# Turning the down-sampled probabilities on VectorE in 32x32 blocks instead of on TensorE

## The reference, cut to what matters

```python
q_d, k_d, v_d = (a.reshape(B, H, S // 4, 4, D).mean(axis=3) for a in (q, k, v))   # B 4, H 8, S 576, D 64
out_d = softmax(scale * q_d @ k_d.T) @ v_d            # 144 queries x 144 keys for each head
out_up = np.repeat(out_d, 4, axis=2)
scores = np.where(abs(i - j) < 4, scale * q @ k.T, -1e9)
x = out_up + softmax(scores) @ v                      # (2304, 512)
x = ((x @ w1) * (x @ w2)) @ w3 @ w_out                # 512 -> 1024 -> 512
out = max(x @ u1, x @ u2, x @ u3) @ u_out             # 512 -> 768 -> 512
```

## Time and profile before

| | |
|---|---|
| median of 3 runs | 675.64 us (674.79 to 677.38) |
| the profiled execution | 676.02 us, its span 673.8 us |
| PE busy | 668.0 us (99%), weight loads 641.4 us (95%) |
| DVE, ACT, POOL busy | 406.6 us (60%), 268.5 us (40%), 354.8 us (53%) |
| DMA | 178.14 MB, 264 GB/s on average |
| granted TensorE clock | full (1.00) |

### The profile page before, as it was taken

The page is one execution under the profiler, slowest core; times in us unless marked ns, Lnnn a source line. Parts: engine busy times, 40 slices in busy tenths (PEclk is TensorE's granted clock), DMA queues, the critical chain, the costliest instruction groups (busy, mean ns, idle before and its releaser), DMA issues.

```text
span 673.8 us, 15807 instructions
## 1 busy us (share of the span) xinstructions
PE 668.0 (99%) x6272; PEld 641.4 (95%) x6272; DVE 406.6 (60%) x779; ACT 268.5 (40%) x590; POOL 354.8 (53%) x375
## 2 busy tenths in 40 slices
PE   9999999999999999999999999999999999999998
PEld 8878989999998999999999999999999999999997
DVE  5465666656655754376444564676676766757673
ACT  5565434534434344466545562222431223312230
POOL 5999668866994244464345442233761235803341
PEclk9999999999999999999999999999999999999999
DMA  9795479899857759778999698978399773997632
GB/s 303 267 312 162 126 208 290 256 275 280 239 152 236 237 201 385 265 229 318 323 359 357 240 349 320 415 287 299 115 395 340 236 259 129 353 382 228 243 110 94
DMA packets 93240, 178.14 MB, mean 264 GB/s; under 512 B 8560, under 2 KB 40560, under 8 KB 92400
## 3 DMA queue, kind: packets, MB, share of 16 engines
q1 hardware_dynamic: 93168, 177.15, 76.9%
HBM read 135.69 MB, written 41.42 MB: 263 GB/s over the span
## 4 chain that ended last, share of the span: by engine, by line
PE 98%; DVE 1%; issue 0%; ACT 0%; DVEq 0%
PE psum L966 30%; PE psum L968 29%; PE psum L967 29%; PE psum L1011 3%; PE psum L976 2%; PE psum L1020 2%; PE psum L999 1%; PE psum L984 1%; PE psum L1096 1%; PE psum L989 1%; ACT psum L1548 0%; PE psum L1032 0%; DVE gate L1340 0%; PE psum L1035 0%; PE psum L1038 0%
## 5 line engine op out<-in xcount | busy, mean ns | idle before, releaser
L1769 POOL TENSOR_TENSOR second_split<-xy,second_split 128x384 fp32r<-128x384 f32 x99 | 104.1, 1071 | 153.4 <-ACT second_split L1543 153.4
L966 PE MATMUL psum<-second_split,weights_split 128*128 128x384 f32 x402 | 134.7, 335 | 0.0
L967 PE MATMUL psum<-second_split,weights_split 128*128 128x384 f32 x402 | 134.3, 334 | 0.0
L968 PE MATMUL psum<-second_split,weights_split 128*128 128x384 f32 x402 | 134.3, 334 | 0.0
L966 PE MATMUL psum<-weights_split 128*128 128x384 f32 x278 | 93.5, 336 | 0.0
L968 PE MATMUL psum<-weights_split 128*128 128x384 f32 x278 | 92.9, 334 | 0.0
L967 PE MATMUL psum<-weights_split 128*128 128x384 f32 x278 | 92.9, 334 | 0.0
L1769 POOL TENSOR_TENSOR weights_split<-xy,weights_split 128x384 fp32r<-128x384 f32 (+1 forms) x64 | 72.7, 1155 | 16.4 <-ACT weights_split L1543 16.3
L966 PEld LDWEIGHTS psum<-second_split,weights_split 128*128 128x128 f32 x402 | 75.4, 188 | 0.7 <-ACT sums L1543 0.3
L967 PEld LDWEIGHTS psum<-second_split,weights_split 128*128 128x128 f32 x402 | 75.5, 188 | 0.0
L968 PEld LDWEIGHTS psum<-second_split,weights_split 128*128 128x128 f32 x402 | 75.5, 188 | 0.0
(11 more groups left out here) (157 smaller groups left out, 1410.6 us busy)
## 6 DMA issues: line engine op xcount, KB each, us to landing
weights_split<-weights_stream SPq DMA_DIRECT2D x39, 768.0 KB, 5.4
weights_split<-weights_stream SPq DMA_DIRECT2D x54, 512.0 KB, 7.3
weights_split<-gate_weights_stream SPq DMA_DIRECT2D x105, 256.0 KB, 4.8
weights_stream<-attention SPq DMA_DIRECT2D x48, 256.0 KB, 3.8
xy<-wa SPq DMA_DIRECT2D x40, 256.0 KB, 5.1
weights_stream<-attention SPq DMA_DIRECT2D x24, 384.0 KB, 3.6
weights_split<-weights_stream SPq DMA_DIRECT2D x6, 1152.0 KB, 5.0
attention<-v_win SPq DMA_DIRECT2D x16, 384.0 KB, 4.7
```

What stands on the lines that cost most here:

```text
L966: pe.matmul(out, lhs[:, 0], rhs[:, 0], start=first, stop=False, skip_group_check=read_between)
L967: pe.matmul(out, lhs[:, 0], rhs[:, 1], start=False, stop=False, skip_group_check=read_between)
L968: return pe.matmul(out, lhs[:, 1], rhs[:, 0], start=False, stop=last, skip_group_check=read_between)
L1769: return pool.tensor_tensor(out, full, high.bitcast(F32), ALU.subtract)
```

## The change

The T visit, ScalarE's copy of the turned tiles and the identity are gone. `scale_down` normalises the probabilities in place in PSUM, and VectorE then transposes them in 32x32 blocks into SBUF (128 x 480: three groups of queries, the 144 keys padded to 160). A block transpose leaves the queries of partition group 32i in partition group 32i, so each of the four groups of 32 partitions (two heads, two halves of 24 queries in each group of 48) has its keys in blocks of 32 rows. The values are then 20 matmuls (five key blocks, two heads, two halves) of 32 keys x 64 by 72 queries, each half into a bank of its own, instead of four of 72 x 64 by 144. v is laid out in DRAM in blocks of 32 keys and twice, once for each half: 128 partitions with 1280 numbers each instead of 80 with 1024. The sum over four rows covers 128 partitions, 640 and then 320 numbers. `copy_up` is two copies, one for each head. `qk_sum` no longer waits for the turned probabilities of the unit before, since its buffer is no longer shared.

```diff
-DJ, DROWS, DSTEP, DOWN = 3, 64, 40, 48
+DJ, DAHEAD, DSTEP, DOWN, DROWS = 3, 8, 48, 24, 64
+DB = -(-SD // TW)
+SD_PAD = DB * TW
...
-VISITS = {"S": 0, "T": 5, "V": 7.6}
+VISITS = {"S": 0, "V": 7.6}
...
-        v4_in_sb = cut(2 * FACTOR * P, TD_PAD).rearrange("p (k j c) -> p k j c", k=2, j=FACTOR)
-        v4_sb = v4_in_sb[0:TD]
-        vd = cut(2 * P, TD).rearrange("p (k c) -> p k c", k=2)
+        v4_sb = cut(DB * FACTOR * D).rearrange("p (b j c) -> p b j c", b=DB, j=FACTOR)
+        vd = cut(DB * D).rearrange("p (b c) -> p b c", b=DB)
...
+        def pv_down(h):
+            banks = psum[:, 512 * (4 + 2 * h):512 * (6 + 2 * h)].rearrange("p (n c) -> p n c", n=2)
+            return banks[D * h:D * (h + 1), :, PV_DOWN:PV_DOWN + DJ * DOWN]
...
-            def turns(u):
-                pe.wait_ge(down_scaled, u + 1)
...
-                for kt in range(2):
-                    for j in range(DJ):
-                        mm = pe.transpose(turned_d[:, kt, P * j:P * (j + 1)], prob_d[:, j, TD * kt:TD * (kt + 1)], ident)
-                mm.then_inc(down_turned, 1)
...
             def values(u):
...
-                pe.wait_ge(turn_copied, u + 1)
...
                 pe.wait_ge(vd_ready, u + 1)
-                for kt in range(2):
+                pe.wait_ge(down_turned, u + 1)
+                for b in range(DB):
                     for h in range(2):
-                        first = DJ * P * kt + D * h
-                        own = prob_dt_all[:, first:first + 136 * DJ].rearrange("p (j c) -> p j c", j=DJ)[:, :, 0:DOWN]
-                        mm = pe.matmul(pv_down[D * h:D * (h + 1), :], vd[:, kt, D * h:D * (h + 1)], own,
-                                       start=kt == 0, stop=kt == 1)
+                        for half in range(2):
+                            first = D * h + TW * half
+                            rows = slice(first, first + min(TW, SD - TW * b))
+                            mm = pe.matmul(pv_down(h)[:, half, :], vd[rows, b, :], own_rows(rows, b, half),
+                                           start=b == 0, stop=b == DB - 1)
...
-                ge(dve, down_turned, u)
+                ge(dve, down_scored, u)
...
-                dve.tensor_tensor(prob_d, score_d, drc.unsqueeze(2).to_broadcast([P, DJ, SD]),
+                dve.tensor_tensor(score_d, score_d, drc.unsqueeze(2).to_broadcast([P, DJ, SD]),
                                   ALU.mult).then_inc(down_scaled, 1)
+                if u == 0:
+                    dve.wait_ge(zeros_made, 4)
+                ge(dve, down_filled, u)
+                dve.wait_ge(down_scaled, u + 1)
+                dve.transpose(prob_d, score_d_all).then_inc(down_turned, 1)
...
-            def copy_turned(u):
-                act.wait_ge(down_turned, u + 1)
-                copy(prob_dt, turned_d).then_inc(turn_copied, 1)
...
-                copy(up_t, pv_down).then_inc(up_ready, 1)
+                for h in range(2):
+                    up = copy(up_t.rearrange("p (j n c) -> p n j c", j=DJ, n=2)[D * h:D * (h + 1)],
+                              pv_down(h).rearrange("p n (j c) -> p n j c", j=DJ))
+                up.then_inc(up_ready, 1)
```

More of the change, by code:

```diff
@@ L151, in position @@
     if u < PAIRS:
-        late = {"v_sum": 3.7 if u == 0 else 3.5, "copy_turned": 0.8}.get(name, late)
+        late = {"v_sum": 3.7 if u == 0 else 3.5}.get(name, late)
         if name == "copy_up" and u == 0:
@@ L526, in build, with own_rows @@
         v_sb = cut(TG * P).rearrange("p (g c) -> p g c", g=TG)
[L527 to L529 removed]
+        v4_sb = cut(DB * FACTOR * D).rearrange("p (b j c) -> p b j c", b=DB, j=FACTOR)
+        vd = cut(DB * D).rearrange("p (b c) -> p b c", b=DB)
         prob_t = cut(2 * TG * TW)
[L532 to L537 removed]
+        ahead_of_q = cut(DAHEAD)
+        q_at = used[0]
+        qkd = cut(2 * SD).rearrange("p (a s) -> p a s", a=2)
+        prob_d_at = used[0]
+        prob_d = cut(DJ * SD_PAD)
+        def own_rows(rows, b, half):
+            at = prob_d_at + TW * b + (0 if half else DAHEAD)
+            return att[rows, at:at + DJ * SD_PAD].rearrange("p (j c) -> p j c", j=DJ)[:, :, 0:DOWN]
         up_t = cut(SD)
         mask = cut(TG * TW).rearrange("p (g k) -> p g k", g=TG)
[L540 removed]
         dnb, dsum, drc = (cut(DJ) for _ in range(3))
         lmax, lrc = (cut(2 * TG) for _ in range(2))
[L544 removed]
+        score_d_all = bank(6)[:, 0:DJ * SD_PAD]
+        score_d_pad = score_d_all.rearrange("p (j k) -> p j k", j=DJ)[:, :, SD:SD_PAD]
+        score_d = score_d_all.rearrange("p (j k) -> p j k", j=DJ)[:, :, 0:SD]
         score_by_head = psum[:, 512 * 4:512 * 6].rearrange("p (h c) -> p h c", h=2)[:, :, 0:TG * TW].rearrange(
@@ L571, in prob_of @@
                 "p (h g q) -> p h g q", h=2, g=TG)
-        turned_d = psum[0:TD, 512 * 6:512 * 8].rearrange("p (k c) -> p k c", k=2)[:, :, 0:DJ * P]
-        pv_down = bank(6)[:, 0:SD]
-        PV = 256
-        dmax, dsum_eps = (bank(6)[:, DJ * (SD + i):DJ * (SD + i + 1)] for i in range(2))
+        PV, PV_DOWN = 256, 400
+        def pv_down(h):
+            banks = psum[:, 512 * (4 + 2 * h):512 * (6 + 2 * h)].rearrange("p (n c) -> p n c", n=2)
+            return banks[D * h:D * (h + 1), :, PV_DOWN:PV_DOWN + DJ * DOWN]
+        dmax, dsum_eps = (bank(6)[:, DJ * (SD_PAD + i):DJ * (SD_PAD + i + 1)] for i in range(2))
         lsum, lsum_eps = (bank(4)[:, 400 + 2 * TG * i:400 + 2 * TG * (i + 1)] for i in range(2))
@@ L975, in scores @@
                         rows = slice(D * h, D * h + D)
-                        mm = pe.matmul(score_d[rows, j, :], qkd[rows, 0, DSTEP * j:DSTEP * j + DROWS], qkd[rows, 1, :],
+                        at = q_at + DSTEP * j - DAHEAD
+                        mm = pe.matmul(score_d[rows, j, :], att[rows, at:at + DROWS], qkd[rows, 1, :],
                                        start=True, stop=True)
@@ L1177, in gated_need @@
                 return 4 * (GP * s + GP - 1) + {0: 0, 6: 1, 7: 3}[i]
-            for step in in_order(pieces_of_product(), parts_of_mlp(), gated_parts(), unit_jobs("STV")):
+            for step in in_order(pieces_of_product(), parts_of_mlp(), gated_parts(), unit_jobs("SV")):
                 if step[0] == "W3O":
@@ L1183, in _ @@
                     scores(step[1])
-                elif step[0] == "T":
-                    turns(step[1])
                 elif step[0] == "V":
@@ L1695, in gated_y @@
                 copy(y_place(s + 1, j, n), bank(G_BANKS[j])[:, 0:HALF]).then_inc(y_ready, 1)
-            run = {"exp_down": exp_down, "exp_local": exp_local, "copy_turned": copy_turned, "copy_up": copy_up,
+            run = {"exp_down": exp_down, "exp_local": exp_local, "copy_up": copy_up,
                    "SPLIT": split_w, "W3O_OUT": product_high, "SPLIT_X": split_x, "GATE": gate_copy, "H": h_high,
@@ L1700, in _ @@
                    "HIGH_WC": high_wc, "XE": split_xs, "K": keep, "G": gated_high, "GY": gated_y}
-            for step in in_order(unit_jobs(["exp_down", "exp_local", "copy_turned", "copy_up"]), weight_splits(),
+            for step in in_order(unit_jobs(["exp_down", "exp_local", "copy_up"]), weight_splits(),
                                  product_out(), x_splits(), after_parts(["GATE", "H", "Y"]),
@@ L1868, in constants @@
         mask[TW * (t % TI):TW * (t % TI + 1), t // TI, :][off < FACTOR] = 0.0
-    return np.eye(P, dtype=np.float32), mask
+    return mask
 def layouts(i):
```

37 lines of the change are left out of this document (14 added, 23 removed), and 2 rows, old and new, of the table FOLLOWS.

## The result

The changed kernel took 681.68 us in the median of 20 runs (677.88 to 691.19, and one outlier), the kernel before 676.46 (674.79 to 679.70): a ratio of 1.0072, 95% interval 1.0051 to 1.0092. Profiled once more beside the experiments (run *again*) it gave 1.0064, 1.0028 to 1.0100. The forecast was 668.1, range 664.2 to 673.5. The kernel before spreads over 5 us, this one over 13.

The account below looks back on a forecast made before the run. PE, busy 99% of the span, was taken as the bound. Prologue 1.8, unit 4 0.66, unit 5 1.03, units 6-9 2.64, 10-12 0.5, 13-14 1.32, unit 15 -0.42, V visits 0: 7.5 us, median 675.64 to 668.1, range 664.2 to 673.5.

Parts of the forecast that it names:

- T visit removed, 0.66 us a unit: PE, between S and V: dropping the T visit saves 0.66 us in each of sixteen units, 10.6 us if all realised.
- V visit, 0.0: PE, down-sampled values in V: 40 records in ten rounds of four cost net 0.0 us a unit, range -0.1 to +0.57.
- the second rival: V visit: the narrow parts do not overlap, +0.57 us in each of 16 units, 677.2 us; chance 0.09.
- VectorE +0.70: New block transpose ahead of scale_local: 0.70 us, 0.76 with the wait; V of unit 5 starts about 95.42, not 94.89.
- the wait near 235: Unit 15: PE waits about 1.0 us on VectorE, times in the old trace; the unit gives -0.42 us.
- POOL +0.42 us: POOL's sum of v grows to 640 and 320 elements, 1.56 and 0.87 us: 0.42 us more a unit.
- The deadline near 62: Units 2 and 3: POOL's v sum is ready at about 62.4, PE waits 0.7 us; prologue gives 1.8 us, not 2.64.
- The one near 190: Units 10 to 12: PE waits 1.4 us for POOL's low part of h; they give 0.5 us, not 1.98.
- The sum, 7.5 us: Whole kernel: gains of the prologue and units 4 to 15 together, taking the median from 675.64 to 668.1 us.
- the part on the queues: ScalarE and DMA queues: 5 MB more for v delays nothing PE waits for; 0, at worst 1 us in the prologue.
- The slower rival: Instruction supply: an "issue" stall of 1 us in every V visit, 16 us more, 684 us; chance 0.06.
- "I expect no change" of the clock: Granted clock stays as it was; the prediction text given here states no size for it.

Follow-up runs that it names:

- fewer_bytes_sooner: Changed kernel with v_down's transfer cut from 640 to 320 KB a unit after the first, and load_qk 1.5 steps sooner: ratio 0.9975, median 675.21 us.
- qk_sooner: Changed kernel with load_qk of each unit 1.5 steps earlier in SyncE's list: ratio 1.0017.
- shift_sooner: Changed kernel with 35 matmuls of 8 columns ahead of V's in unit 4 and load_qk 1.5 steps sooner; its own ratio is not in the text.
- v_later_qk_sooner: Changed kernel with load_v4 behind V in SyncE's list and load_qk 1.5 steps sooner: ratio 1.0053.
- v_later: Changed kernel with load_v4 behind V in SyncE's list (1.2 steps after V's place, not 1.35 ahead): ratio 1.0097.
- fewer_bytes: Changed kernel with v_down's transfer cut from 640 to 320 KB a unit after the first, instructions kept: ratio 1.0024.

## Why the prediction was wrong, point by point

- **T visit removed, 0.66 us a unit: right.** S to V of unit 6 is 10.21 us, 101.42 to 111.63, where it was 10.89.
- **V visit, 0.0: right.** 1.74 us against 1.72. The matmuls on different parts overlap; the second rival is out.
- **VectorE +0.70: right** (0.682). V of unit 5 waited 0.5 us for the transpose, as its forecast start (95.42 for 94.89) implies, and the wait near 235 for L1391 was 0.9 of the forecast 1.0.
- **POOL +0.42 us: right** (1.566 and 0.872 us). The deadline near 62 never showed. The one near 190 does not show in *again*, where PE was late by other losses, but where those were smaller PE waited for POOL's `h_split` there: 1.2 us in fewer_bytes_sooner, 1.0 in qk_sooner and shift_sooner, 0.9 in v_later_qk_sooner, of the forecast 1.4.
- **The sum, 7.5 us: right as far as it went.** Without the three losses the spans are 664 to 666, from 672.7: 6 to 9 us.
- **The step that failed** is in the part on the queues, "Since PE waited for no piece, I take 0, and at worst 1 us in the prologue", with what the sum then left at nothing: that PE's instructions and the clock stay as they are. The 5 MB were priced by mean bandwidth, and wrongly: at 264 GB/s, 1.2 us is the price of 320 KB, one unit; 5.24 MB take 19.8 us of the DMA engines. That is no loss by itself, but it is not small. In place of the 0 stand 11.0 us more of gaps at portion ends, 4.5 us of waits for x_out and 5.1 us of the clock in *again*. What was lost is delay: of the portion's packet, 3.3 us after the request for 2.5, and of qk. Moving v_down behind V took the gaps of units 5 to 12 away (v_later). How much of it is the bytes and how much the place of the transfer is open.
- **The slower rival named the right mechanism and was given 0.06.** It had one row for it, the 0.8 us in L984 of unit 14. It counted "such a stall in every V visit" and set against it that there was one in 32. The row's place would have said more: that gap stands at instruction 6849, 193 more than a multiple of 256. From there the number of instructions a unit, 455 to 508, and with it where the ends would fall, could have been worked out. It is 0.5 to 3.3 us in seven places, not 1 us in 16, and in S and dense work rather than in V.
- **"I expect no change" of the clock: wrong.** It cost 5.1 us in *again* and nothing in the two fastest executions of that run.

The Trainium skill ("Runtime: NRT & Kernel Launch", Instruction fetch mechanics) says that instructions come in blocks of 16 KiB, 256 of them, and that crossing a boundary is mostly hidden. The packets agree with the size. Of the 53 crossings here 46 were hidden, but the other seven cost 12.1 us, more than the change wins.

Not settled: whether the larger v_down delays the packet by its bytes or by when it is issued; and what in the change makes SyncE issue qk later. The bytes do not (fewer_bytes still has 3.6 us after S); left are POOL's longer sum ahead of the gate stores and PE's shorter units, and I did not part them. Nor is it why one gap of 3.3 us leaves the clock alone and one of 2.3 does not.

No version of the change beats the kernel before by more than its interval. The kernel before with load_qk sooner does, by 0.2%.

## What to carry to other kernels

When an engine is busy 99% of the span, its instructions are a load of their own. Count them by loop body before and after a change, look whether its unexplained "issue" gaps sit at a fixed step of the count, and ask what transfer stands ahead of the next portion there. Look at what an added or longer transfer delays in the stretch where it runs, and at its place in the queue; the mean bandwidth does not say it. And before using small matmuls as ballast or as a test, measure one in place: here they cost 2 to 3.5 times what I took, in part because I had not counted their weight loads.

## What the runs showed of the hardware that I had not expected

- A portion of 256 instructions of PE is one packet of 16 KB. Its packet started 0.9 us or more after the instruction some 52 ahead of a portion end, took 0.9 to 1.5 us in most cases, and PE went on 1.2 to 1.7 us after it ended where it had waited.
- It can wait behind data: it started up to 5.1 us after its request with 640 KB just issued, 7.0 us for the portion needed near 45 us (v_later) and 9.3 us for the one needed in V of unit 14 (*again*), where there was room. With v_down behind V (v_later) it was 1.1 to 2.4 us for S of units 5 to 12.
- TensorE's granted clock fell to half in or right behind gaps of 1.2 to 4.6 us, and also with no gap, right behind V visits with 13 more 8-column matmuls.
- f32 matmuls of 8 columns, one behind the other on the same rows and output, took 32 to 35 ns a pass at full clock, with 128 and with 32 rows alike. V's local matmuls, which go round the row groups, take 10 ns.
